# Two-tile up products that stream high and low rows together, and no turn of gathered rows left to TensorE

## The reference

```python
x = attention(q, k, v)                    # 4 x 8 heads, 576 tokens, window 64
x = (sigmoid(x @ w_gate) * (x @ w_val)) @ w_out        # 2304 x 512, hidden 1536
logits = x @ r_gate
noisy = logits + log1p(exp(x @ r_noise)) * noise
top2 = the two largest of 8 experts for each token, weights by softmax
for e in range(8):
    for k in range(2):
        mask = top2[:, k] == e
        h = np.maximum(x[mask] @ w1[e], 0.0)           # 512 -> 1024
        out[mask] += top2_w[mask, k, None] * (h @ w2[e])   # 1024 -> 512
```

## Time and profile before

| | |
|---|---|
| median of three runs | 974.71 us (974.69 to 976.02) |
| the profiled execution | 974.4 us, of which its span 972.5 us |
| PE busy | 963.2 us (99%), 6467 matmuls |
| DVE busy | 516.2 us (53%) |
| ACT busy | 372.1 us (38%) |
| POOL busy | 424.5 us (44%) |
| transfers | 113.64 MB, mean 117 GB/s |
| mean granted clock of TensorE | 0.998 |

### The profile page before, as it was taken

The page is one execution under the profiler, slowest core; times in us unless marked ns, Lnnn a source line. Parts: engine busy times, 40 slices in busy tenths (PEclk is TensorE's granted clock), DMA queues, the critical chain, the costliest instruction groups (busy, mean ns, idle before and its releaser), DMA issues.

```text
span 972.5 us, 17622 instructions
## 1 busy us (share of the span) xinstructions
PE 963.2 (99%) x6467; PEld 847.9 (87%) x6467; DVE 516.2 (53%) x1285; ACT 372.1 (38%) x892; POOL 424.5 (44%) x417
## 2 busy tenths in 40 slices
PE   9999999999999999999999999999999999999997
PEld 7998888888888888888999899898998989898995
DVE  6565576765757576574546633444443434444430
ACT  6553343433333343422344423343434334343411
POOL 4882224242332434232215453664828284664402
PEclk9999999999999999999999999999999999999999
DMA  6756333343533325232134163672736465473503
GB/s 227 233 173 165 119 110 108 96 138 97 142 106 125 99 75 152 76 100 87 44 121 133 30 156 79 169 161 84 156 77 146 100 151 129 118 163 75 98 3 52
DMA packets 85335, 113.64 MB, mean 117 GB/s; under 512 B 20800, under 2 KB 48448, under 8 KB 85248
## 3 DMA queue, kind: packets, MB, share of 16 engines
q1 hardware_dynamic: 71376, 85.18, 30.0%
q0 software_dynamic: 13584, 27.05, 13.9%
q10 hardware_dynamic: 288, 0.26, 0.1%
HBM read 83.69 MB, written 28.77 MB: 116 GB/s over the span
## 4 chain that ended last, share of the span: by engine, by line
PE 98%; ACT 1%; DVE 0%; issue 0%; POOL 0%; POOLq 0%; DVEq 0%
PE bank L1129 22%; PE bank L1113 22%; PE bank L1018 16%; PE bank L1041 16%; PE bank L1024 11%; PE bank L1022 5%; PE bank L998 2%; PE bank L936 2%; PE bank L1136 1%; PE bank L1067 1%; PE bank L1077 0%; PE bank L954 0%; ACT arena L1268 0%; PE bank L1097 0%; POOL out L816 0%
## 5 line engine op out<-in xcount | busy, mean ns | idle before, releaser
L1024 PE MATMUL bank<-xr,wr 128*128 128x256 f32 x864 | 242.6, 281 | 0.0
L1018 PE MATMUL bank<-xr,wr 128*128 128x512 f32 x672 | 239.9, 397 | 0.0
L1113 PE MATMUL bank<-wr 128*128 128x256 f32 (+1 forms) x1536 | 223.4, 306 | 0.3 <-DVE wr L1748 0.3
L1113 PEld LDWEIGHTS bank<-wr 128*128 128x128 f32 x1536 | 221.2, 190 | 2.0 <-DVE wr L1748 0.7
L798 POOL DMA_INDIRECT arena<-x_rows,shared x128 | 139.8, 1092 | 131.2 <-DVE v_nat L1735 88.4
L763 POOL TENSOR_TENSOR hr<-arena,hr 128x256 fp32r<-128x256 f32 x84 | 62.0, 738 | 263.5 <-ACT hr L1319 263.5
L1041 PE MATMUL bank<-wr,hr 128*128 128x512 f32 x648 | 170.6, 398 | 0.0
L1024 PEld LDWEIGHTS bank<-xr,wr 128*128 128x128 f32 x864 | 163.6, 189 | 3.5
L1018 PEld LDWEIGHTS bank<-xr,wr 128*128 128x128 f32 x672 | 126.2, 188 | 30.2
L1041 PEld LDWEIGHTS bank<-wr,hr 128*128 128x128 f32 x648 | 114.0, 188 | 23.7 <-issue 0.6
L1129 PE MATMUL bank<-wr 128*128 128x512 f32 (+1 forms) x576 | 132.6, 390 | 0.0
(11 more groups left out here) (161 smaller groups left out, 1013.6 us busy)
## 6 DMA issues: line engine op xcount, KB each, us to landing
arena<-moe_w SPq DMA_DIRECT2D x36, 512.0 KB, 3.7
arena<-moe_w SPq DMA_DIRECT2D x112, 128.0 KB, 3.4
p_rows<-arena SPq DMA_DIRECT2D x28, 256.0 KB, 2.0
v_nat<-p_rows SPq DMA_DIRECT2D x112, 64.0 KB, 2.0
arena<-gv SPq DMA_DIRECT2D x12, 512.0 KB, 4.5
out<-zeros POOLq DMA_DIRECT2D x20, 256.0 KB, 2.8
x_rows<-arena SPq DMA_DIRECT2D x9, 512.0 KB, 3.9
arena<-k SPq DMA_DIRECT2D x17, 256.0 KB, 4.2
```

The lines of the kernel that those rows point to most:

```text
L1018: pe.matmul(ps_g[m].rearrange("p (a n) -> p a n", a=2), gv_w[:, f, m, kk], xr[:, g % 2, :, kk], start=(kk == 0), stop=False, skip_group_ch ...
L1024: mm = pe.matmul(ps_g[m][:, 0:GT], gv_w[:, f, 2 + m, kk], xr[:, g % 2, 0, kk], start=False, stop=(kk == KC - 1), skip_group_check=True)
L1113: mm = pe.matmul(ps_h[u % 2][:, 0:n], w1_r[e % 2][:, a, kk, f * P:(f + 1) * P], xT[p][:, b, kk, 0:n], start=(kk + x == 0), stop=(kk == KC ...
```

## The change

It has five parts.

1. `SQUARES` is gone. Every tile is gathered in quarters and turned by DVE. The five `turn_g` on TensorE go, and five `turn_rows` on DVE come: n = 0 in step 103, n = 1 in step 104, n = 2 in step 106, n = 6 and n = 7 inside the half (1,0).
2. The parts of turned tile n = 2 move: `FIRST_ROWS = [LAST - 4, LAST - 3, LAST - 1]` puts `xt_high(2)` and `xt_low(2)` into step 107 instead of 106, behind `h_high` and `h_low`.
3. The tables of quarter numbers grow. `tab_q_first` holds two experts (8 transfers instead of 4) and is needed in step 100 instead of 103, before the first gather. A new `tab_q_next` (4 transfers, ahead of `tab` and `tab_q` in SP's list) serves gathers 6 and 7. `tab_q` holds eight experts instead of seven. POOL's `gather(7)` moves ahead of `scatter(1)`. The first four weight loads of expert 0 become 16.
4. In the p = 1 half of every expert but expert 1, `up` issues one product of 512 columns and one of 256 where it issued three of 256. DVE adds the two halves of the bank into `gate[:, f % 2]` (`add_cols`), and `relu` and `hidden_low` read from there. `up` of step f then waits for `add_cols` of step f - 2.
5. For the last group `choose_first` is split, and `hidden_low(0, 0, 5)` stands behind its first three instructions instead of behind all eight.

```diff
-    SQUARES = 1
+    FIRST_ROWS = [LAST - 4, LAST - 3, LAST - 1]
...
+        def wide_up(e, p):
+            return p == 1 and e != AHEAD - 1
...
+            for j in range(4):
+                sp.dma_start(tab_q_next[j * Q4:(j + 1) * Q4].rearrange("p b n w -> p b (n w)"),
+                             by_quarter[:, :, 0, 2 * HEAD:2 * TILES]).then_inc(tab_q_next_in, 16)
             sp.dma_start(tab[:]...
...
+                if n == 0:
+                    pool.wait_ge(quarters_first, 1)
+                if n == AHEAD * HEAD:
+                    pool.wait_ge(quarters_next, 1)
...
             gather(6)
+            gather(7)
             scatter(1)
-            gather(7)
...
-                if u >= 2:
+                if wide_up(e, p) and f >= 2:
+                    pe.wait_ge(cols_added, wide_no(e, f) - 1)
+                elif u >= 2:
                     pe.wait_ge(ht_lo, u - 1)
...
+                    if wide_up(e, p):
+                        pe.matmul(ps_h[u % 2].rearrange("p (a n) -> p a n", a=2), w1_r[e % 2][:, 0, kk, f * P:(f + 1) * P],
+                                  xT[p][:, :, kk, 0:n], start=(kk == 0), stop=False, skip_group_check=True)
+                        mm = pe.matmul(ps_h[u % 2][:, 0:n], w1_r[e % 2][:, 1, kk, f * P:(f + 1) * P], xT[p][:, 0, kk, 0:n],
+                                       start=False, stop=(kk == KC - 1), skip_group_check=True)
+                        continue
...
-                if LAST - 4 <= s < LAST - 1:
-                    turn_g(s - (LAST - 4))
...
-                if f in (4, 6):
-                    turn_g(f // 2 + 4)
...
+            def add_cols(e, f):
+                u = F2C * half_no(e, 1) + f
+                dve.wait_ge(up_done, u + 1)
+                dve.wait_ge(ht_lo, u - 1)
+                dve.tensor_reduce(gate[:, f % 2], ps_h[u % 2].rearrange("p (a n) -> p n a", a=2), AX.X, ALU.add).then_inc(cols_added, 1)
...
                 if s == LAST - 5:
-                    dve.wait_ge(tab_q_first_in, 16 * 4)
...
+                    turn_rows(0)
+                if s in FIRST_ROWS:
+                    xt_low(FIRST_ROWS.index(s))
+                if s == LAST - 4:
+                    turn_rows(1)
+                if s == LAST - 2:
+                    turn_rows(2)
...
+            dve.wait_ge(tab_q_next_in, 16 * 4)
+            to_quarters(tab_q_next[:]...).then_inc(quarters_next, 1)
             for f in range(F2C):
                 hidden_low(1, 0, f)
...
+                if f == 3:
+                    turn_rows(6)
+                if f == 4:
+                    xt_low(6)
+                if f == 5:
+                    turn_rows(7)
+                    xt_low(7)
```

More of the change, by code:

```diff
@@ L380, in attention_two_moe_program @@
         ORDER = [0, 1, 2, 5, 6, 7, 3, 4, 8, 9] + list(range(AHEAD * TILES, ALL))
-        def turned_at(n):
-            return x_t if squared(n) else ps_xt.rearrange("p (k m) -> p k m", k=KC)
         def turn_no(m):
             return ORDER.index(m)
-        def squared(n):
-            return ORDER[n] // TILES >= SQUARES
         def loads(q):
-            return 16 * sum(4 if i // UNITS >= SQUARES and i % UNITS < KC else 1 for i in range(q % 4, q + 1, 4))
+            return 16 * sum(4 if i % UNITS < KC else 1 for i in range(q % 4, q + 1, 4))
         def gathers(n):
-            return 16 * sum(4 if squared(i) else 1 for i in range(n % 2, n + 1, 2))
+            return 64 * ((n - n % 2) // 2 + 1)
         def is_early(m):
@@ L414, in wide, with wide_no @@
             return FC <= c < LAST - FC
+        def wide_up(e, p):
+            return p == 1 and e != AHEAD - 1
+        def wide_no(e, f):
+            return F2C * (e if e < AHEAD - 1 else e - 1) + f
         def row_of(c):
@@ L524, in _ @@
         def _(sp):
+            by_quarter = places.rearrange("(b c e n) w -> c b e (n w)", b=4, c=Q4, e=NE)
             def load_k(t):
@@ L665, in _ @@
                                      ).then_inc(tab_first_in, 16)
[L666 to L669 removed]
+                    for e in range(AHEAD):
+                        for j in range(4):
+                            sp.dma_start(tab_q_first[j * Q4:(j + 1) * Q4, e].rearrange("p b n w -> p b (n w)"),
+                                         by_quarter[:, :, e, 0:2 * HEAD]).then_inc(tab_q_first_in, 16)
                     for n in range(4, UNITS):
@@ L1089, in rank_rows @@
                 pe.matmul(ps_rank, tri[:], chosen[:], start=False, stop=True, skip_group_check=True).then_inc(ranked, 1)
-            def turn_g(n):
-                pe.wait_ge(gathered[n % 2], gathers(n))
-                if n:
-                    pe.wait_ge(xt_lo, n)
-                pe.nop(nofuse=True)
-                for kk in range(KC):
-                    mm = pe.transpose(ps_xt[:, kk * P:(kk + 1) * P], x_g[:, n % 2, kk * P:(kk + 1) * P], ident[:])
-                mm.then_inc(xt_turned, 1)
             def up(e, p, f):
@@ L1393, in relu @@
                 n = HR if p == 0 else LT
-                act.activation(hT[p][:, 0, f, 0:n], ps_h[u % 2][:, 0:n], ACT.Relu).then_inc(ht_hi, 1)
+                act.activation(hT[p][:, 0, f, 0:n], gate[:, f % 2] if wide_up(e, p) else ps_h[u % 2][:, 0:n], ACT.Relu
+                               ).then_inc(ht_hi, 1)
             def rows_out(e, a):
@@ L1480, in _ @@
                 relu(1, 0, f)
-                if f in (4, 6):
-                    xt_high(f // 2 + 4)
+                if f in (3, 5):
+                    xt_high(6 + (f - 3) // 2)
             for f in range(F2C):
@@ L1666, in choose_first, with add_noise @@
             def choose_first(g):
+                add_noise(g)
+                choose(L[:], marks[:, 0], top[:, 0])
+            def add_noise(g):
                 dve.wait_ge(soft, 3 * g + 2)
@@ L1832, in _ @@
             hidden_low(0, 0, 4)
-            choose_first(GROUPS - 1)
+            add_noise(GROUPS - 1)
             hidden_low(0, 0, 5)
+            choose(L[:], marks[:, 0], top[:, 0])
             choose_second(GROUPS - 1)
@@ L1850, in _ @@
                     to_quarters(tab_q[:].rearrange("p b e n w -> p (b e n) w")[:, :, 0]).then_inc(quarters_done, 1)
-                if f in (4, 6):
-                    xt_low(f // 2 + 4)
+                if f == 3:
[5 more added lines that the diff above has]
+                    xt_low(7)
+            add_cols(0, 0)
             for f in range(F2C):
+                if f + 1 < F2C:
+                    add_cols(0, f + 1)
                 hidden_low(0, 1, f)
@@ L1872, in _ @@
             for e in range(AHEAD, NE):
-                for p in range(2):
-                    for f in range(F2C):
-                        hidden_low(e, p, f)
-                        if p == 0 and f < KC:
-                            low(e, KC + f)
+                for f in range(F2C):
+                    hidden_low(e, 0, f)
+                    if f < KC:
+                        low(e, KC + f)
+                add_cols(e, 0)
+                for f in range(F2C):
+                    if f + 1 < F2C:
+                        add_cols(e, f + 1)
+                    hidden_low(e, 1, f)
                 for a in range(TILES):
```

78 lines of the change are left out of this document (38 added, 40 removed).

## The result

The changed kernel takes **976.83 us** (median of 14 executions, 975.51 to 980.37); the kernel before, beside it, 974.98 (14 executions, 974.42 to 976.82). The ratio is 1.0018 with a 95% interval of 1.0011 to 1.0025: 1.8 us slower, between 1.1 and 2.4. I had forecast 974.3, 0.4 us less, and gave a slower kernel a chance of 0.18. The time lies in my range, but it moved the other way.

What follows compares the result with a forecast made beforehand. PE's chain, 98% of the span, was taken as the bound. Terms +1.5 - 0.3 - 0.9 + 1.3 - 2.0 = -0.4 us on 974.4 gave 974.0; the median 0.3 above made 974.3 us, range 971.8 to 977.2.

Steps and rivals of the forecast that it cites:

- the wait for gather 7: Ahead of `up(0,1,0)`: TensorE waits behind gather 7's landing and the transpose of n = 7; +1.3 us, bounds 0 and +4.2.
- the distance A: Stretch from `up(1,0,0)` to `down(0,3)`; predicted +0.1 us from two turns less, the gather wait and a seventh of the pairing.
- The pairing: Paired `up` products in the p = 1 halves of seven experts: 0.009 us saved per triple, 224 triples, -2.0 us.
- First term: Ahead of `up(0,0,0)`: DVE's added transposes make `xt_low(2)` late and TensorE idles 2.4 us; net +1.5 us.
- rival B: Before expert 0: `xt_low(2)` no later than TensorE, so its three turns are gained too; 970.6 to 971.8 us, chance 0.13.
- The split choose: Ahead of `up(0,0,7)`: `hidden_low(0,0,5)` comes about 1 us earlier and TensorE's 0.34 us wait goes; -0.3 us.
- The two turns: Inside half (1,0): two pieces of about 0.44 us leave TensorE's chain; -0.9 us if nothing replaces them.
- the 1.2 us in hand: Half (1,0): gather 6 has 1.2 us to spare, and the whole `tab_q` about as much.
- I cost it at nothing: Gather 8, half (0,1): lands while DVE has 0.3 us to spare per step, hidden by `up(0,1,3)` and `up(0,1,4)`; no cost.
- Rival E: Paired `up` products: columns alone set the distance, so the merge saves nothing; 976.3 us, chance 0.06.
- C: Transpose of n = 7: transfers hold half (0,1) if landing exceeds 4.7 us; at 9.2 us +4.2, 977.2 us, chance 0.10.
- D: Idle time ahead of `up(0,0,0)` drops TensorE's clock, doubling the products behind it; +3.4 us, 977.7 us, chance 0.07.

Runs made afterwards that it cites:

- Experiment 5: Changed kernel with the transpose of n = 2 and `xt_low(2)` earlier on DVE, `xt_high(2)` ahead of `h_high(107)` on ACT: 974.47 us, ratio 0.9997.
- experiment 3: Kernel before with the paired products and the split choose, all turns of expert 0 left on TensorE: 972.63 us, ratio 0.9977.
- experiment 9: Changed kernel with the edits of Experiment 5 and experiment 7, `tab_q` multiplication behind `xt_low(6)`, `weights(GROUPS - 2)` behind `h_low(107)`: 972.03 us, ratio 0.9966.
- experiment 2: Changed kernel without the paired products: all `up` products narrow, `add_cols` left out: 978.05 us, ratio 1.0037.
- experiment 6: Changed kernel with 18 products on zeros, `idle(18)`, on TensorE ahead of `up(0,0,0)`: 977.38 us, ratio 1.0025.
- experiment 10: Changed kernel with 10 products on zeros, `idle(10)`, on TensorE ahead of `up(0,0,0)`: 976.70 us, ratio 1.0013.
- experiment 4: Changed kernel with SP issuing expert 1's weights from unit 4 on only once gather 7 has landed: 976.22 us, ratio 1.0014.
- experiment 7: Changed kernel with the edit of experiment 4 and the transpose of n = 8 at f = 4 instead of f = 1 in half (0,1): 975.31 us, ratio 1.0002.
- experiment 12: Changed kernel with `idle(10)`, 10 products on zeros, ahead of both `up(0,0,0)` and `up(0,1,f)`: 977.39 us, ratio 1.0025.

## Why the prediction was wrong

The step that failed is the wait for gather 7, a term of the third part: put at +1.3 us, it measured +2.9. It turned the forecast loss of 0.1 us in the distance A into one of 1.9. The pairing, put at -2.0, gave 1.3. Together they turned -0.4 into +1.9.

**First term, right.** +1.5 predicted, +1.62 measured, by the mechanism named: the transposes buy nothing, `xt_low(2)` is last. The place is right step by step too: shifted by the 4.0 us that lie ahead, `h_rows(107)` was due at 525.5 and came at 525.46, the end of `xt_low(2)` was due at 527.6 and came at 527.52. Experiment 5 shows that the place in DVE's list is the cause, not DVE's load: the three turns do fit. What I held against rival B (no air on DVE) was wrong as a general claim, since a few instructions in another order, on DVE and on ACT, took 1.8 us off the first distance.

**The split choose, right in place and sign, too small in size.** -0.3 predicted, -0.64 in experiment 3 alone: I took the idle time of a row for the cost from start to start.

**The gathers, the step that failed.** I had +1.3 for the wait and -0.9 for the two turns; A rose by 1.90 although pairing took 0.1 off it. The two turns did give 0.9: in experiment 9, with the waits gone, `up(0,1,0)` starts 16.00 us after `up(1,0,0)`, before it was 16.89. In the changed kernel it is 18.93, so the wait cost 2.9 us, not 1.3. The landing was right (6.3 predicted, 6.36 measured), and so was the rest behind it (2.6; 582.73 less 580.05 is 2.68). Late was the start: on the shifted clock (+5.1) I had POOL's first issue at 563.4 and it came at 564.70. I had DVE multiply as soon as it was free, and POOL issue at once; the table came 0.7 us after DVE stood waiting, and POOL took 0.78 from the end of the multiplication. Every such microsecond goes through. That is 1.3 of the 1.6 us that I missed. The rest are small readings: 0.1 between landing and transpose, 0.1 behind it, and 0.1 because TensorE is ready at 16.00 and not at 574.8 - 558.67 = 16.13. The wait isn't one number: by the same distance, less 16.00, the waits of this half come to 2.5, 2.4 and 2.8 us in the profiles of experiments 2, 5 and 6 and to 4.1 in that of 10, which have the same lists there. In those, 0.4, 0.7, 0.4 and 0.9 us stand ahead of `up(1,0,6)`: `hidden_low(1,0,4)` comes late, behind the multiplication of `tab_q`, which waits for its loads, and the transpose of n = 6. The changed kernel's profile has no such wait. So the 1.2 us in hand that I gave gather 6 and `tab_q` were not always there; experiment 9 puts that multiplication later.

I had also looked at gathers 6 and 7 alone. What limits this stretch is POOL's list: six more issues of 1.26 us (eight quarters where two gathers stood), so that once gather 7 is in time gather 8 is not (experiment 4). "I cost it at nothing" holds only while gather 7 is late.

**The pairing, right in mechanism, too large.** -2.0 predicted, -1.3 measured, 1.15 us / 192 triples = 6.0 ns instead of 9. My lower bound was 1.4. The source was a difference of four readings of `gate_val`, a neighbour, not this product. Yet 12.2 ns stand in experiments 4 and 7 (2.35 / 192), so the rhythm isn't fixed. The Trainium skill (TensorE: Matmul & The Clock Gate, section Back-to-back issue gap) would have 2.5 ns per product less, by a formula that it gives for isolated products and not for a stream of weight loads and products as here; neither rhythm agrees. Rival E is refuted: by it nothing would have come.

**The rivals.** C named the right place and the wrong cause: not a late landing, but a late start. D's mechanism is real in a part of the executions: I had argued from a clock that fell 3.3 us after the last product; it fell behind gaps of 2.14 and 2.16 us too, and 1.55 us were lost there, not the 3.4 of my text. In the changed kernel's profile it fell behind neither gap, so the 1.9 us of the table are explained without D. In the median D may hold some 0.9 us, by my estimate from the two kinds of executions (976.83 less 975.9). No run isolates that share. The Trainium skill (TensorE: Matmul & The Clock Gate, section HAM oscillation — how this bites in real kernels) describes the same for waits on transfers: they drop the clock, and the next products start slow. The runs here agree, with two additions: the waits of 2.14 and 2.16 us ended with VectorE and not with a transfer, and the same wait does it only sometimes. My sentence "no wait for `add_cols`" was right, as was "no wait ahead of `up(0,0,7)`".

In sum, the forecast missed by 2.3 us on the trace: 1.8 of the distance A, 0.55 of the pairing in experts 2 to 7, 0.1 of the first term and 0.1 in places where I had nothing, less 0.2 of the choose.

## What to carry to other kernels

When work moves from one engine to another, count what it adds to every list on the way, the queue that issues its transfers above all. Here a turn of 0.44 us on TensorE went, and in its place GpSimd issued four gathers of 1.26 us each instead of one, behind a table, a multiplication and a hand-over of 0.8 us, and the stretch had no room for them. The move paid only after the lists around it were rewritten (experiment 9, 3.0 us), and most of that was to be had from the other parts alone (experiment 3, 2.1 us); the two intervals overlap. Look for the second wait behind the one that you remove: it is often the next item of the same list.

## What the runs showed of the hardware

- TensorE's granted clock fell to 0.50 (1.2 GHz) behind a gap of 2.14, 2.16 and 2.69 us in three profiles (experiments 4, 7, 10), and stayed at 1.00 (2.4 GHz) behind 2.15 and 2.51 (changed kernel) and 2.14 (experiment 2). In experiments 4 and 7 it fell only after work had resumed; in the gap of 5.60 us it fell inside it. The price was 1.55 us, and 1.5 in experiment 10 (12.90 us from up(0,1,0) to down(0,3), in the changed kernel 11.37). In the changed kernel's profile it also stood at 0.50 behind a gap of 2.13 us in the attention, and the first gated product came 3.6 us late.
- The same paired triple recurs in one of two rhythms, 512-column products of 399 or 394 ns on average over the stretch of experts 2 to 7, 1.2 us over six experts. It can change within an execution: in experiment 12 the half (0,1) takes 11.18 us to down(0,3), against 11.37, while down(1,0) to down(7,0) is at the slower rhythm's 327.57. What chooses is open.
- POOL's issue of a gather comes 0.78 us after the end of the DVE instruction that releases it, for the first quarter of gather 6 in all eleven traces that have `tab_q_next` (changed kernel 564.70 less 563.92, experiment 4 562.68 less 561.90, experiment 2 560.65 less 559.87).
- A product of `idle` (128x128 on zeros) takes 0.219 us at full clock and leaves two records, where the products around it leave one each. Counting records as products halves its price.
